# Adding the small constant to a head's softmax sums on ScalarE in place of VectorE

## The reference, cut to what matters

```python
scores = scale * q @ k.T + decay            # masked above the diagonal
attn = exp(scores - max(scores))
attn = attn / (sum(attn) + 1e-9)
x = attn @ v                                # 2304 tokens x 512
h = x @ w_in;  g = h * sigmoid(1.702 * h);  x2 = g @ w_out      # w_in 512x2048
# soft mixture: 32 slots over all tokens, 8 small experts, mixed back to the tokens
```

## Time and profile before

| | us |
|---|---|
| median of 3 runs | 756.2 (756.04 to 756.49) |
| the profiled execution's own time | 757.33 |
| its span, first to last instruction | 755.5 |
| PE busy | 703.7 (93%) |
| DVE busy | 448.8 (59%) |
| ACT busy | 436.8 (58%) |
| POOL busy | 438.6 (58%) |

### The profile page before, as it was taken

How to read it: one execution, slowest core, us unless ns; L and a number is a source line. 1 busy time by engine, 2 the same in 40 slices (tenths; PEclk the granted TensorE clock), 3 DMA queues, 4 the chain that set the end, 5 groups by cost and what they waited for, 6 DMA issues and landing times.

```text
span 755.5 us, 15808 instructions
## 1 busy us (share of the span) xinstructions
PE 703.7 (93%) x5923; PEld 666.7 (88%) x5923; DVE 448.8 (59%) x1255; ACT 436.8 (58%) x1031; POOL 438.6 (58%) x511
## 2 busy tenths in 40 slices
PE   3899998999999799999999999999999999998993
PEld 3888888999899799999998899999999999995662
DVE  5898867777777556676666466767542432224323
ACT  4788875576657566666676675757555344311112
POOL 3355667585758766676768675858476477520000
PEclk9999999999999999999999999999999999998997
DMA  4334554544645353374541635463214354598966
GB/s 105 108 93 108 141 102 122 123 97 120 124 122 121 90 123 104 105 138 125 129 119 69 134 96 123 122 138 93 70 60 137 126 189 147 177 396 346 389 283 250
DMA packets 102651, 108.85 MB, mean 144 GB/s; under 512 B 62832, under 2 KB 72048, under 8 KB 100528
## 3 DMA queue, kind: packets, MB, share of 16 engines
q1 hardware_dynamic: 102576, 107.85, 50.1%
HBM read 103.03 MB, written 4.79 MB: 143 GB/s over the span
## 4 chain that ended last, share of the span: by engine, by line
PE 71%; DVE 12%; ACT 7%; issue 3%; POOL 3%; DMA 1%; SPq 0%; DVEq 0%; POOLq 0%
PE mb L1260 47%; PE yb L1111 5%; PE zb L1131 5%; PE xb L1157 4%; PE mb L1312 2%; DVE prob L888 2%; ACT prob L733 2%; DVE sums_e L881 2%; DVE ptl L894 2%; PE xb L1091 2%; PE yb L1351 1%; POOL xl L677 1%; DMA stage<-in_moe_w_in 1%; DVE kl L850 1%; DVE qs L846 1%
## 5 line engine op out<-in xcount | busy, mean ns | idle before, releaser
L1260 PE MATMUL mb<-xh,wih 128*128 128x288 f32 x512 | 157.7, 308 | 9.4 <-DVE hid L975 5.2
L1260 PE MATMUL mb<-gh,woh 128*128 128x288 f32 x512 | 156.8, 306 | 5.6 <-DVE x2t L982 5.3
L1260 PE MATMUL mb<-gh,wol 128*128 128x288 f32 x512 | 151.1, 295 | 0.0
L1260 PE MATMUL mb<-xh,wil 128*128 128x288 f32 x512 | 151.1, 295 | 0.0
L1260 PE MATMUL mb<-gl,woh 128*128 128x288 f32 x512 | 151.0, 295 | 0.0
L1260 PE MATMUL mb<-xl,wih 128*128 128x288 f32 x512 | 150.9, 295 | 0.0
L687 POOL TENSOR_TENSOR gl<-hid,gh 128x288 fp32r<-128x288 f32 x128 | 103.2, 811 | 36.1 <-ACT gh L774 35.3
L975 DVE SCALAR_TENSOR_TENSOR hid<-gate,mb 128x288 f32<-128x288 f32 x128 | 57.7, 451 | 107.7 <-ACT gate L780 107.2
L733 ACT ACTIVATE prob<-prob,m_row 64x576 f32<-64x576 f32 (+4 forms) x160 | 96.4, 604 | 32.6 <-DVE m_row L874 31.6
L704 POOL TENSOR_TENSOR wil<-stage,wih 128x512 fp32r<-128x512 f32 x64 | 81.8, 1288 | 48.9 <-ACT wih L719 48.9
L704 POOL TENSOR_TENSOR wol<-stage,woh 128x512 fp32r<-128x512 f32 x64 | 82.7, 1293 | 44.5 <-ACT woh L719 44.5
(11 more groups left out here) (201 smaller groups left out, 1472.6 us busy)
## 6 DMA issues: line engine op xcount, KB each, us to landing
stage<-in_moe_w_in SPq DMA_DIRECT2D x64, 256.0 KB, 3.7
stage<-in_moe_w_out SPq DMA_DIRECT2D x64, 256.0 KB, 2.8
ring_a<-in_moe_w SPq DMA_DIRECT2D x16, 1024.0 KB, 6.8
ring_b<-in_moe_w SPq DMA_DIRECT2D x14, 1024.0 KB, 13.0
qk_in<-in_q SPq DMA_DIRECT2D x32, 144.0 KB, 2.9
qk_in<-in_k SPq DMA_DIRECT2D x32, 144.0 KB, 3.3
v_in<-in_v SPq DMA_DIRECT2D x32, 128.0 KB, 3.0
result<-ring_a SPq DMA_DIRECT2D x16, 256.0 KB, 3.1
```

The source lines that it names most:

```text
L1260: ins = mm(bank[:, 0:HALF], a[:, t, P * (j % 4):P * (j % 4) + P], x[:, t, cols], start=(i == 0), stop=(i == 11))
```

## The change

The addition moves to ScalarE, right behind the head's last exponential, with a wait for that exponential's accumulator to have landed. VectorE's norm no longer waits for the exponentials itself, but for the semaphore `sum_eps`, which ScalarE now raises. The reciprocal and the multiplications stay as they are.

```diff
@@ scalar, step "score"
                         nc.scalar.activation(prob[0:r, par, POFF[i]:POFF[i] + w], prob[0:r, par, POFF[i]:POFF[i] + w],
                                              ACT.Exp, bias=m_row[0:r, par, i:i + 1], scale=-1.0,
                                              accum_out=sums[0:r, par, i:i + 1]).then_inc(expd, 1)
+                    if st[2] == 3:
+                        act.wait_ge(expd, b * 40 + 5 * s + QT)
+                        nc.scalar.activation(sums_e[:, par, :], sums[:, par, :], ACT.Copy, bias=EPS).then_inc(sum_eps, 1)
@@ vector, step "norm"
                     n = b * 8 + s
-                    dve.wait_ge(expd, 5 * n + 5)
-                    nc.vector.tensor_scalar(sums_e[:, par, :], sums[:, par, :], EPS, None, ALU.add).then_inc(sum_eps, 1)
                     dve.wait_ge(sum_eps, n + 1)
                     nc.vector.reciprocal(rsum[:, par, :], sums_e[:, par, :]).then_inc(sum_inv, 1)
                     dve.wait_ge(sum_inv, n + 1)
```

## The result

| | before | changed |
|---|---|---|
| median, us | 756.35 (756.04 to 757.28, 4 runs) | 751.95 (751.38 to 753.14, 4 runs) |
| ratio | | 0.9943, 95% interval 0.9927 to 0.9959 |
| the profiled execution, its span | 757.33, 755.5 | 751.85, 749.9 |

A later series gave 751.5 us and 0.994 (0.992 to 0.996).

The account below looks back on a forecast made before the run. TensorE, busy 93%, was taken as the bound, waiting where GpSimd stalls VectorE's add; -1.44 - 0.96 - 0.20 + 0.24 = -2.36 us from 756.2 gave 753.8 us, range 752.0 to 756.6.

Parts of the forecast that it names:

- The stall moves to the first multiplication, and 0.48 us of the path is saved where it is felt: VectorE's norm: first L888 stalls instead of the add; 0.48 us saved at each of three TensorE waits inside batches, 1.44 us.
- no TensorE wait follows in the head at 169 us: Long add at 169.50 us: TensorE's own work covers it before any wait follows, so nothing is gained.
- 0.96 us at the two batch ends: Long adds at 243.15 and 401.97 us, where batches meet: 0.48 us saved at each.
- L740's earlier start may matter at 251 us, but the wait at 264 takes it back: First batch end: ScalarE's L740 some 0.8 us earlier may shorten TensorE's first wait; TensorE then waits longer at 264.
- +0.24 us for the hand-over in batch 0: Batch 0's eight heads: passing the sums from ScalarE to VectorE costs +0.03 us a head.
- -0.2 at 95 us: Between batch 0 and 1, the add took 0.47 us on the chain; 0.2 us taken as saved.
- ScalarE's queue costs nothing: Woven heads: copy and wait delay ScalarE's queue by about 0.3 us, costed at nothing thanks to idle time before L740.
- the rivals: Four alternatives: stall moves whole (756.4, chance 0.15), hand-over dearer (754.8, 0.12), stall vanishes (750.0, 0.10), ScalarE late (slower, 0.08).
- The one in which the stall vanishes: VectorE's norm: the stall was the add's own or finds an earlier pause; 6.2 us saved, 750.0 us, chance 0.10.

Follow-up runs that it names:

- e2: Changed kernel with VectorE's old 128x5 add put back before the reciprocal as a dummy into an unused buffer; 756.05 us, ratio 0.9993.
- e3: Changed kernel with a second 128x5 reciprocal on VectorE before the real one, into an unused buffer; 752.5 us, ratio 0.9947.
- e7: Kernel before with twelve unread 128-column matmuls put into TensorE's longest wait, behind the head at 113 us; 754.65 us, ratio 0.9987.
- e5: Kernel before, VectorE's add untouched, plus ScalarE's copy and its wait as a dummy into an unused buffer; 756.51 us, ratio 1.0006.
- e1: Changed kernel with the add of 1e-9 left out on every engine, VectorE waiting for the exponentials itself; 751.27 us, ratio 0.9938.
- e9: Changed kernel run once more without further change, in a later series; 751.5 us, ratio to before 0.994.
- e4: Changed kernel, but ScalarE's multiplication of tile 4 waits for VectorE's first multiplication, not the reciprocal; 754.9 us, ratio 0.9981.
- e10: Changed kernel, but GpSimd waits for VectorE's four multiplications before the gap of work ahead of its mask step; later series, 749.79 us, ratio 0.9914.
- e6: Kernel before with VectorE's add written as an instruction with two tensor inputs in SBUF, ScalarE taking no part; 757.02 us, ratio 1.0011.
- e11: Kernel before, VectorE keeping its add, with only GpSimd's wait for the four multiplications added, as in e10; 753.42 us, ratio 0.996.
- e8: Same kernel as e10 against the kernel before, run in the earlier series; 751.47 us, ratio 0.9938.

## Why the forecast was right, and where it fell short

- *The stall moves to the first multiplication, and 0.48 us of the path is saved where it is felt*: right. The three waits inside batches shrank by 0.48 each, and e2 against e3 shows that it is the kind of instruction that counts. The moved stall is smaller than I said: 735 ns in the mean and 23.5 us in all, for 980 and 31. In the head at 206 us the add stood for 3.60 us, and the first multiplication, which comes to the port later, for 3.20; 128x384 took 2.2 us of the stall as well (15.4 us, from 13.2). I had said that no TensorE wait follows in the head at 169 us; a short one did (at 172.93 in the kernel before), and 0.2 us came from it.
- *The sum went wrong by a missing term*: behind the longest of these waits the kernel before lost TensorE's clock, and the change, by making that wait 1.51 us, kept it. It is worth 1.57 us in the trace and 1.54 by e7. I had read that wait's length, and not the granted clock behind it, which stands at 0.50 in the trace of the kernel before. With it, three waits at 0.48, the 0.2, and the 0.96 of the batch ends, the forecast of 2.4 becomes 4.2; with the 0.3 that the next point leaves of the 0.96, it is 3.5.
- *0.96 us at the two batch ends*: right in sign, loose in size. Kernels with the old instruction in place (e5 to e7) take 71.5 us for the first of them where the profile of before took 72.4, and those with it gone (changed, e1, e3, e9) 71.1 to 71.6: about 0.3 us that can be told. The stretch with the second takes 158.5 to 159.7 us in the former (157.9 in the profile of before) and 157.1 to 157.7 in the latter. The second TensorE wait there hangs on weight transfers and varies from 0.3 to 2.2 us between profiles, so one profile of each does not size it.
- *L740's earlier start may matter at 251 us, but the wait at 264 takes it back*: half right. Tile 4 starts 0.86 us earlier, for the 0.8 I gave, but VectorE's split behind it takes 0.32 us longer, so that the first wait shrank by 0.53 only. I had no term for that split. The wait at 264 did not take the rest back in this profile: it went from 2.19 to 1.52.
- *+0.24 us for the hand-over in batch 0, and -0.2 at 95 us*: the price of the hand-over was right, its effect was not. From the end of the accumulator's read to the reciprocal it is now 0.27 us, for 0.24 before; the timeline of ScalarE and VectorE in the changed kernel:

```profile
39.09 0.19 ACT L733 ACTIVATION_READ_ACCUMULATOR prob<-prob,m_row 128x1 f32 x1
...
39.31 0.21 ACT L738 ACTIVATE sums_e<-sums 128x5 f32<-128x5 f32 x1
...
39.55 0.19 DVE L884 RECIPROCAL rsum<-sums_e 128x5 f32<-128x5 f32 x1 [0.77 <-ACT sums_e L738]
```

  TensorE waits 0.42 us for it in place of 0.40, and the heads take the same time. A TensorE wait is not yet a bound: in e1 halving it changed no head's length. What does bind batch 0 I have not tested, beyond e4's tile 4. The gain at 95 us did not come either (that wait is 0.62 us, for 0.56). The two terms, +0.24 and -0.20, cancelled in the sum by luck.
- *ScalarE's queue costs nothing*: right, by e5 (1.0006). The copy takes 208 ns, where I took 190.

Of the rivals, none happened. The one in which the stall vanishes (750.0) is as near in time as the forecast, 1.95 us off for 1.85, but the stall is there, 23.5 us of the first multiplication. It is the traces that tell them apart, not the time.

## What to carry to other kernels

Where a tiny instruction shows a mean far above its shortest, ask what it waits for in the other engine's timeline, and whether the next instruction will wait for the same; only what lies behind the stall's end is saved. Keep port-taking instructions out of the place between a stall's end and the work that others wait for, and let the engine that fills the port wait at the point where the other's short burst is due (e10). Then look for the next place where the two engines meet: work that comes earlier on one of them can collide anew, as the split at the batch ends did. Behind each longer wait of TensorE read the granted clock too: here 1.99 us of waiting had another 1.57 behind it.

## What the runs showed of the hardware

- VectorE's 128x5 add waited through up to four GpSimd instructions that followed each other without a pause, up to 3.60 us. In the kernel before it stood for more than 0.25 us in 15 heads, and each time it ended 0.03 us behind a GpSimd instruction that the next one did not follow at once: the pause was 1.7 us or more in ten of them and 0.03 to 0.08 us in five (0.04 in rows 7, where the next one begins at 327.26). A reciprocal of the same five columns took 187 to 193 ns in all 32 heads of both kernels.
- TensorE's granted clock fell to 0.50 for some 3 us behind waits of 1.85 to 1.99 us at 118 us (before, e2, e5, e6, e11), and not behind 1.49 to 1.51 at the same place (changed, e1, e3, e4, e8 to e10). The length of the wait does not decide alone: 2.66 us gave 0.52 at 249 us and 1.00 at 408 us in one execution (e4), and 2.19 at 264 us in the kernel before cost no clock.
- The batch ends can cost clock too, which the profile of the kernel before does not show. Behind the first wait there, of 1.83 to 1.85 us in the kernels with the old instruction, the clock stayed at 1.00 at both ends in before and e7 (and in e2, at 1.71 us), fell to 0.50 at the second end in e5 and e6, and at both in e11; behind 1.29 to 1.34 us (changed, e1, e3, e8, e9, e10) it fell at neither. The mean granted clock of all fast runs points the same way: 0.986 over 63 of the kernel before, 0.991 over 22 of the changed kernel, e1, e3 and e9. On a span of some 750 us these means give an estimate of 3 to 4 us lost to the clock, of which some may lie in the last 190 us. So the 1.57 us may be less than what the change saves by the clock in the mean of many executions; no run here takes that apart. The busy times of e5 over 410 to 413 us, columns as above:

```profile
410.00:413.00 3.00, 3.00 (x15) 2.98 (x15) 1.06 (x2) 0.00 (x0) 3.00 (x3) 0.50 0.03 4
```
